# Attention probabilities times values cut in three parts of two key tiles instead of two parts of three

## The chip, the cores and the metric

The kernel runs on one core of a Trainium2 chip. The metric is the device time of one execution in microseconds. Runs of the kernel before gave 668.71, 668.14 and 669.58 us, median 668.71 us.

## The reference

The program is an attention with a hash mask, a Fourier mixing with a feed-forward block, and a gated convolution. The change touches the attention alone, and its last product:

```python
# q, k, v: 2 batches, 8 heads, 768 rows, head dimension 64; proj: 64 x 6
q_bucket = sum(((q @ proj) > 0) * powers);  k_bucket = sum(((k @ proj) > 0) * powers)
scores = where(q_bucket == k_bucket, q @ k.T / sqrt(64), -1e9)
attn = exp(scores - rowmax) / (rowsum + 1e-9)
x = attn @ v                          # <- the change is in the order of this product
u = x + real(fft(fft(x, axis=1), axis=2))
y = u + relu(norm(u) @ w_ch1) @ w_ch2
out = (sigmoid(causal_conv(y)) * (y @ w_val)) @ w_out
```

## The kernel before

The attention takes the first two fifths of the execution, to about 260 us. It works on pairs of heads, eight of them (`NP`), numbered i. A pair has twelve slots (`SLOTS`), one for each tile of 128 query rows: slots 0 to 5 hold the six tiles of the pair's first head, slots 6 to 11 those of its second. Pair 0 and pair 7 are written out; pairs 1 to 6 are the body of a hardware loop; a further round, numbered 8, has no scores and finishes what pair 7 left. Every engine follows an order written out by hand, and semaphores tie the orders together. Nothing is scheduled at run time.

In each slot, TensorE (function `pair`, lines 1286 to 1326) does the following, in this order:

- `scores` (line 1243): four matmuls of 384 columns write one query tile's scores into two PSUM banks. They wait (line 1239) until ScalarE has done the exponential of the tile two slots earlier, because only two such buffers exist.
- "P": six transposes (line 1307) of the probabilities of the tile two slots earlier, in two halves P0 and P1. Each half goes to one of three scratch banks in turn, and waits until the use three before it has been drained.
- in some slots a task that prepares the operands of a later head: B in slots 1 and 7 (line 1199), C0 in 2 and 8, C1 in 4 and 10 (line 1205), or "O" in slots 3 and 6, three transposes of a finished output (line 1315).
- in the slots that the table `PV_SLOTS` (line 241) lists, one part of the product with the values, `p_times_v` (lines 1246 to 1263).

The product has two halves g of the query rows for each pair, and each half sums over six key tiles kt into PSUM bank 7, both heads side by side: head 0 writes partitions 0 to 63 and head 1 partitions 64 to 127. Each (kt, head) is one float32 matmul in the program and two MATMUL records, each with its own weight load, in the trace, so one key tile has four records. Before the first part of a half TensorE waits for the transposed probabilities, for the values and for the copy of the bank's previous contents (`outT_copied`). After the last part it signals `pv_done`; ScalarE then copies the bank (line 686), later drains of the transposed probabilities may overwrite them, and the next values are loaded.

On VectorE a slot has the minimum of the new scores (line 927), a drain of half of the transposes (line 342) and the preparation's drains (lines 915 to 920). On ScalarE it has the exponential (line 676), the other drain (line 342), the rounding of the next operands, and the copy of the output (line 686).

Of the kernel before, what the change touches and what calls it, by code (L numbers as in the profile page):

```python
# [6 lines left out]
def attention_fft_ffn_gate_kernel(nc, qT, kT, v, proj, w_ch1, w_ch2, w_val, conv_wT, w_out,  # L7
# [27 lines left out]
    HT = T // 2  # L35
# [16 lines left out]
    with ctx:  # L52
# [172 lines left out]
        def need(eng, semaphore, value):  # L225

            if not isinstance(value, int) or value > 0:
                eng.wait_ge(semaphore, value)
# [9 lines left out]
        OUT_SLOT = {3: 0, 6: 1}  # L238

        P1_BY_ACT = (9,)  # L240
        PV_SLOTS = {11: (0, 0), 1: (0, 1), 2: (1, 0), 4: (1, 1)}
        uses = []
        for s in range(SLOTS):
            uses += [(s, "P0"), (s, "P1")]
# [45 lines left out]
        def wait_drained(eng, i, use):  # L290

            need(eng, scratch_free[bank_of(i, use)], use_number(i, use))
# [900 lines left out]
        def _(pe):  # L1193
# [17 lines left out]
            def prepare(i, use):  # L1211
                h, nxt = head_of_task(i, use)
                wait_free(i, use)
                if use[1] == "B":

                    need(pe, q_scaled, operands(i + nxt, h) + 1)
                    op = bits(i, use, h)
                else:
                    if use[1] == "C0":

                        of_head = range(6) if use[0] < 6 else range(6, SLOTS)
                        wait_drained(pe, i, (0 if isinstance(i, int) and i < 0 else
                                             next(x for x in of_head if "B" in PREPARE.get(x, [])), "B"))
                    op = buckets(i, use)
                op.then_inc(scratch_full[bank_of(i, use)], 1)
# [21 lines left out]
            def p_times_v(i, g, part):  # L1247

                if part == 0:

                    tile = T + HT * (g + 1) - 1
                    j, s = (i, tile + 2) if tile + 2 < SLOTS else (i + 1, tile + 2 - SLOTS)
                    wait_drained(pe, j, (s, "P0"))
                    wait_drained(pe, j, (s, "P1"))
                    need(pe, v_loaded, 32 * (i + 1))

                    need(pe, outT_copied, i * 2 + g)
                for kt in range(HT * part, HT * part + HT):
                    for h in range(2):
                        op = pe.matmul(PS[h * D:(h + 1) * D, 7, 0:HALF], v_in[:, h, kt, :],  # L1260
                                       probT[h][:, kt, g * HALF:(g + 1) * HALF], start=(kt == 0), stop=(kt == T - 1))
                if part == 1:
                    op.then_inc(pv_done, 1)

            def sequence_step(b, t, blocks):
# [23 lines left out]
            def pair(i, last):  # L1289
                first = isinstance(i, int) and i == 0  # L1290
                for s in range(SLOTS):
# [5 lines left out]
                    for use in slot_tasks(i, s, last):  # L1297
# [19 lines left out]
                        else:  # L1317
                            prepare(i, use)
                    if s in PV_SLOTS:
                        g, part = PV_SLOTS[s]  # L1320
                        if s == SLOTS - 1:
                            if last < 2:
                                p_times_v(i, g, part)
                        elif not first:
                            p_times_v(i - 1, g, part)
# [325 lines left out]
```

## Time and profile before

| | |
|---|---|
| median of three runs | 668.71 us |
| the profiled execution's own time | 668.71 us |
| its span, first to last instruction | 667.0 us |
| TensorE matmul busy | 633.6 us, 95% |
| TensorE weight load busy | 512.9 us, 77% |
| VectorE busy | 362.5 us, 54% |
| ScalarE busy | 304.6 us, 46% |
| GpSimd busy | 250.3 us, 38% |
| matmuls of the product with the values (line 1260) | 384 records, mean 494 ns, 69.0 us |

Matmuls are pipelined: one begins long before the one ahead of it has ended, so durations of single matmuls can't be added. What a step costs is read from the starts of the steps: from the start of its first matmul to the start of the first matmul of the next.

### The profile page before, as it was taken

The page shows a single profiled execution, that of the slowest core. Times are in us where ns is not written, and L with a number is a line of the kernel's source. Part 1 is how long each engine was busy: PE and PEld are TensorE (multiplying, and loading weights), DVE is VectorE, ACT ScalarE, POOL GpSimd, SP SyncE. Part 2 cuts the span into 40 slices and gives each one's busy share as a digit, 9 for nine tenths or more (in the row PEclk, how much of TensorE's full clock was granted, in tenths as well). Part 3 has the DMA queues.
Part 4 walks back from the last instruction along what each step waited for, and adds up shares of the span by engine and source line. Part 5 has one row for each costly group of instructions (what it writes and reads, how often), then busy time and mean ns, then how long its engine had stood idle before and what let it go on. Part 6 is the DMA issues. An engine that isn't in the chain of part 4 may idle for free.

```text
span 667.0 us, 11293 instructions
## 1 busy us (share of the span) xinstructions
PE 633.6 (95%) x3810; PEld 512.9 (77%) x3810; DVE 362.5 (54%) x599; ACT 304.6 (46%) x586; POOL 250.3 (38%) x202
## 2 busy tenths in 40 slices
PE   2999999999999999889999999999999999996998
PEld 1667666766767676888888888889888888885786
DVE  2878796877878786986111111116333333279720
ACT  2877676868677673465222222233222222251132
POOL 6643333335343243744233333326444444343140
PEclk9999999999999999989999999999999999998899
DMA  5822231323222000100222222511222221000102
GB/s 126 247 76 77 66 94 48 105 73 104 71 71 71 1 24 1 49 1 1 63 64 63 63 63 63 189 64 32 63 63 63 63 63 47 1 0 1 63 32 94
DMA packets 34263, 42.08 MB, mean 63 GB/s; under 512 B 3521, under 2 KB 22209, under 8 KB 34241
## 3 DMA queue, kind: packets, MB, share of 16 engines
q1 hardware_dynamic: 32512, 37.77, 19.4%
q0 software_dynamic: 1728, 4.02, 2.3%
q8 instruction: 14, 0.23, 0.2%
q14 instruction: 9, 0.07, 0.0%
HBM read 38.63 MB, written 3.15 MB: 63 GB/s over the span
## 4 chain that ended last, share of the span: by engine, by line
PE 82%; DVE 11%; issue 3%; POOL 2%; ACT 1%; DMA 1%; SPq 0%; DVEq 0%; POOLq 0%; ACTq 0%
PE banks L1457 20%; PE banks L1445 20%; PE banks L1260 10%; PE banks L1243 10%; PE banks L1307 7%; PE banks L1552 5%; PE banks L1199 2%; DVE row_min L927 2%; PE banks L1536 2%; DVE x_then_u_then_gate L1135 2%; PE banks L1380 2%; PE banks L1432 1%; DVE x_then_u_then_gate L1132 1%; DVE k_b L920 1%; PE banks L1283 1%
## 5 line engine op out<-in xcount | busy, mean ns | idle before, releaser
L1122 DVE SCALAR_TENSOR_TENSOR h_lo<-banks,h_hi 128x512 fp32r<-128x512 f32 x64 | 35.5, 558 | 180.8 <-ACT h_hi L825 180.8
L927 DVE TENSOR_REDUCE row_min<-banks 128x1 f32<-128x768 f32 x96 | 91.2, 956 | 42.2 <-PE banks L1243 41.7
L676 ACT ACTIVATE prob<-banks,row_min 128x768 f32<-128x768 f32 x96 | 87.1, 907 | 30.3 <-DVE row_min L927 30.3
L1445 PE MATMUL banks<-unT_hi,w_hi 128*128 128x512 f32 (+1 forms) x256 | 86.3, 337 | 0.0
L1445 PE MATMUL banks<-unT_hi,w_lo 128*128 128x512 f32 (+1 forms) x256 | 86.2, 337 | 0.0
L1445 PE MATMUL banks<-unT_lo,w_hi 128*128 128x512 f32 (+1 forms) x256 | 86.1, 336 | 0.0
L1307 PE MATMUL banks<-ident,prob 128*128 128x128 f32 x576 | 79.6, 274 | 2.2 <-DVE probT L342 1.3
L1307 PEld LDWEIGHTS banks<-ident,prob 128*128 128x128 f32 x576 | 67.2, 140 | 9.8 <-ACT probT L342 2.6
L563 POOL TENSOR_TENSOR w_lo<-w_stage,w_hi 128x512 fp32r<-128x512 f32 x32 | 43.5, 1361 | 83.0 <-ACT w_hi L741 83.0
L501 POOL TENSOR_TENSOR k_b<-k_raw,k_a 64x768 fp32r<-64x768 f32 x16 | 29.1, 1820 | 120.5 <-ACT k_a L659 120.5
L825 ACT ACTIVATE h_hi<-banks 128x512 fp32r<-128x512 f32 x64 | 31.2, 491 | 89.5 <-PE banks L1445 89.5
L568 POOL TENSOR_TENSOR w_lo<-w_stage,w_hi 128x512 fp32r<-128x512 f32 x32 | 41.6, 1302 | 79.4 <-ACT w_hi L746 79.4
L1260 PE MATMUL banks<-probT,v_in 128*64 128x384 f32 x384 | 69.0, 494 | 0.7 <-ACT outT L686 0.7
L1457 PE MATMUL banks<-h_hi,w_lo 128*128 128x512 f32 (+1 forms) x256 | 65.9, 339 | 0.0
L1457 PE MATMUL banks<-h_hi,w_hi 128*128 128x512 f32 (+1 forms) x256 | 65.9, 339 | 0.0
L1457 PE MATMUL banks<-h_lo,w_hi 128*128 128x512 f32 (+1 forms) x256 | 65.3, 337 | 0.0
L746 ACT CAST w_hi<-w_stage 128x512 fp32r<-128x512 f32 x32 | 19.9, 622 | 98.4 <-PE banks L1457 98.4
L1243 PE MATMUL banks<-k_a,q_a 128*128 128x384 f32 x192 | 59.1, 389 | 6.0 <-ACT prob L676 3.1
L342 ACT COPY probT<-banks 128x384 f32<-128x384 f32 x104 | 49.0, 481 | 32.2 <-PE banks L1307 31.2
L1135 DVE SCALAR_TENSOR_TENSOR x_then_u_then_gate<-x2T,taps,x_then_u_then_gate (+1 forms) x64 | 56.3, 879 | 5.3 <-DVE x_then_u_then_gate L1135 2.7
L1243 PEld LDWEIGHTS banks<-k_a,q_a 128*128 128x128 f32 x192 | 29.3, 191 | 34.1 <-ACT prob L676 21.2
L1445 PEld LDWEIGHTS banks<-unT_hi,w_hi 128*128 128x128 f32 x256 | 48.1, 188 | 6.7
(148 smaller groups left out, 1223.5 us busy)
## 6 DMA issues: line engine op xcount, KB each, us to landing
w_stage<-in_moe_w_ch SPq DMA_DIRECT2D x64, 256.0 KB, 2.9
q_raw<-in_q SPq DMA_DIRECT2D x32, 192.0 KB, 3.3
k_raw<-in_k SPq DMA_DIRECT2D x32, 192.0 KB, 3.6
v_in<-in_v SPq DMA_DIRECT2D x16, 192.0 KB, 2.4
out<-y_out SPq DMA_DIRECT2D x12, 256.0 KB, 2.0
seq_tables_sb<-in_dft POOLq DMA_DIRECT2D x6, 386.0 KB, 3.7
wvo_stage<-in_moe_w_val SPq DMA_DIRECT2D x1, 1024.0 KB, 5.3
wvo_stage<-in_moe_w_out SPq DMA_DIRECT2D x1, 1024.0 KB, 7.8
```

Source lines behind the costliest of these rows:

```text
L342: copy(dst, src).then_inc(scratch_free[bank_of(i, use)], 1)
L563: pool.tensor_tensor(w1_lo[:, slot, :, :], w1_stage[:, slot, :, :], w1_hi[:, slot, :, :].bitcast(F32), ALU.subtract).then_inc(w1_lo_done, 1)
L568: pool.tensor_tensor(w2_lo[:, slot, :], w2_stage[:, slot, :], w2_hi[:, slot, :].bitcast(F32), ALU.subtract).then_inc(w2_lo_done, 1)
L676: act.activation(prob[s % 2][:, :, :], s_tile(s), ACT.Exp, bias=row_min[:, s:s + 1], scale=-1.0, accum_out=row_sum[:, s:s + 1]).then_inc(e ...
L927: dve.tensor_reduce(row_min[:, s:s + 1], s_tile(s), AX.XY, ALU.min).then_inc(min_ready, 1)
L1122: dve.scalar_tensor_tensor(out=h_lo[:, slot, at:at + size], in0=h_bank[c], scalar=0.0, in1=h_hi[:, slot, at:at + size].bitcast(F32), op0=A ...
L1135: dve.scalar_tensor_tensor(out=dst, in0=src, scalar=weight, in1=dst, op0=ALU.mult, op1=ALU.add).then_inc(conv_step, 1)
L1243: op = pe.matmul(s_tile(s)[:, c, :], lhs[:, rows], rhs[:, c * HALF:(c + 1) * HALF], start=start, stop=not start)
L1260: op = pe.matmul(PS[h * D:(h + 1) * D, 7, 0:HALF], v_in[:, h, kt, :], probT[h][:, kt, g * HALF:(g + 1) * HALF], start=(kt == 0), stop=(kt ...
L1307: op = pe.transpose(bank[:, j * P:(j + 1) * P], prob[tile % 2][:, c, j * P:(j + 1) * P], ident[:, :])
L1445: op = pe.matmul(h_bank[c], w_[:, slot, kb, :], x_[:, kb, at:at + size], start=(kb == 0 and m == 0), stop=(kb == KB - 1 and m == 2))
L1457: op = pe.matmul(acc(d, c), w_[:, slot, cols], h_[:, slot, at:at + size], start=False, stop=last, skip_group_check=True)
```

## The change

The table gives each half of the product three slots instead of two, and each part two key tiles (eight records) instead of three (twelve). The first part of a half and its last one are in the slots they were in before (11 and 1 for half 0, 2 and 4 for half 1); the middle part is in slot 0 or slot 3. For each pair the first part runs in slot 11 and the rest in the slots 0 to 4 of the next round.

```diff
-        PV_SLOTS = {11: (0, 0), 1: (0, 1), 2: (1, 0), 4: (1, 1)}
+        PV_SLOTS = {11: (0, 0), 0: (0, 1), 1: (0, 2), 2: (1, 0), 3: (1, 1), 4: (1, 2)}
...
-                for kt in range(HT * part, HT * part + HT):
+                for kt in (2 * part, 2 * part + 1):
                     for h in range(2):
                         op = pe.matmul(PS[h * D:(h + 1) * D, 7, 0:HALF], v_in[:, h, kt, :],
                                        probT[h][:, kt, g * HALF:(g + 1) * HALF], start=(kt == 0), stop=(kt == T - 1))
-                if part == 1:
+                if part == 2:
                     op.then_inc(pv_done, 1)
```

## Rows read from the trace of the kernel before

**Rows 1.** The page: PE's busy line, and the chain that ended last.

```profile
PE 633.6 (95%) x3810; PEld 512.9 (77%) x3810; DVE 362.5 (54%) x599; ACT 304.6 (46%) x586; POOL 250.3 (38%) x202
...
PE 82%; DVE 11%; issue 3%; POOL 2%; ACT 1%; DMA 1%; SPq 0%; DVEq 0%; POOLq 0%; ACTq 0%
```

**Rows 2.** The waits: who waited for whom, us in total, times, longest.

```profile
PEld banks L1243 <- ACT prob L676: 21.2, 40, 1.0
```

**Rows 3.** The timeline, PE alone: start us, us, operation, count, [idle before].

```profile
150.85 0.62 PE L1243 MATMUL banks<-k_a,q_a 128*128 128x384 f32 x2
...
152.51 0.61 PE L1243 MATMUL banks<-k_a,q_a 128*128 128x384 f32 x2
...
154.47 0.62 PE L1243 MATMUL banks<-k_a,q_a 128*128 128x384 f32 x2
...
156.65 0.62 PE L1243 MATMUL banks<-k_a,q_a 128*128 128x384 f32 x2 [0.37 <-ACT prob L676]
...
157.46 0.82 PE L1307 MATMUL banks<-ident,prob 128*128 128x128 f32 x6
158.21 2.16 PE L1260 MATMUL banks<-probT,v_in 128*64 128x384 f32 x12
160.29 0.62 PE L1243 MATMUL banks<-k_a,q_a 128*128 128x384 f32 x2
...
161.10 0.82 PE L1307 MATMUL banks<-ident,prob 128*128 128x128 f32 x6
161.67 0.60 PE L1243 MATMUL banks<-k_a,q_a 128*128 128x384 f32 x2
...
162.46 0.82 PE L1307 MATMUL banks<-ident,prob 128*128 128x128 f32 x6
...
166.08 0.62 PE L1243 MATMUL banks<-k_a,q_a 128*128 128x384 f32 x2
...
171.36 0.49 PE L1315 MATMUL banks<-ident,outT 128*128 128x128 f32 x3
171.60 0.60 PE L1243 MATMUL banks<-k_a,q_a 128*128 128x384 f32 x2
...
180.88 0.62 PE L1243 MATMUL banks<-k_a,q_a 128*128 128x384 f32 x2
```

**Rows 4.** The timeline, weight loads of one part of the product (slot 11).

```profile
158.20 0.20 PEld L1260 LDWEIGHTS banks<-probT,v_in 128*64 128x64 f32 x4 [0.17 <-issue]
...
158.58 0.14 PEld L1260 LDWEIGHTS banks<-probT,v_in 128*64 128x64 f32 x2 [0.18 <-issue]
...
158.90 0.14 PEld L1260 LDWEIGHTS banks<-probT,v_in 128*64 128x64 f32 x2 [0.18 <-issue]
```

**Rows 5.** The timeline at the attention's end, where no scores remain.

```profile
247.32 2.16 PE L1260 MATMUL banks<-probT,v_in 128*64 128x384 f32 x12
...
251.00 2.16 PE L1260 MATMUL banks<-probT,v_in 128*64 128x384 f32 x12
...
255.91 0.55 PE L1315 MATMUL banks<-ident,outT 128*128 128x128 f32 x3
...
256.39 2.16 PE L1260 MATMUL banks<-probT,v_in 128*64 128x384 f32 x12
```

**Rows 6.** The timelines of DVE and ACT, slots 0, 1 and 5.

```profile
161.30 0.96 DVE L927 TENSOR_REDUCE row_min<-banks 128x1 f32<-128x768 f32 x1 [1.22 <-PE banks L1243]
...
176.43 0.96 DVE L927 TENSOR_REDUCE row_min<-banks 128x1 f32<-128x768 f32 x1 [0.90 <-PE banks L1243]
...
166.33 0.48 ACT L686 COPY outT<-banks 128x384 f32<-128x384 f32 x1
```

**Rows 7.** Windows: length, busy by engine (PE, PEld, DVE, ACT, POOL), clock, DMA share, GB/s.

```profile
287.90:291.30 3.40, 1.59 (x13) 1.34 (x12) 2.70 (x9) 3.40 (x9) 0.94 (x2) 1.00 0.00 0
291.30:294.70 3.40, 3.40 (x18) 3.40 (x17) 2.41 (x9) 1.19 (x3) 0.25 (x1) 0.50 0.00 0
...
612.20:622.40 10.20, 6.24 (x14) 4.46 (x15) 9.95 (x14) 1.66 (x2) 4.08 (x2) 0.50 0.00 0
```

## The prediction

> **What bounds the kernel now.** I read the page's first part and the chain of waits first: PE is busy for 95% of the span and carries 82% of the chain that ended last [rows 1]. The reader should ask next whether that holds inside the attention, where the change is. The total of waits says nearly: the only large wait of PE there is for ScalarE's exponential, 21.2 us in 40 waits of the weight load [rows 2], much of it hidden behind matmuls still running.
>
> Then I laid PE's timeline out by slots, for one pair in the steady loop [rows 3]. Scores of slot 8 start at 150.85 and those of the next pair's slot 8 at 180.88, so a pair takes 30.03 us. Slot 0 has scores and transposes alone and takes 161.67 - 160.29 = 1.38 us; that is what PE needs when nothing is late. Slot 9 has the same work and takes 154.47 - 152.51 = 1.96 us, so 0.58 us of waiting; slot 10 has the one matmul of C1 besides and takes 156.65 - 154.47 = 2.18 us, with 0.37 us of plain idle time at its end. Together they exceed 2 x 1.38 by 1.38 us, C1's matmul included, and that is the upper bound of PE's waiting in a pair. From slot 11 to slot 4, where the parts of the product are, PE runs on its own work: slot 11 takes 3.64 us, and its steps, priced below, add up to 3.64. So there an instruction added to PE, or a gap between two kinds of instruction, lengthens the pair by its whole length, unless slots 9 and 10 give it back.
>
> **The change, part by part.** No matmul is added or removed: 384 records before and after. What changes is how often PE enters and leaves a part of the product, and which slots are long.
>
> *The price of one part.* The part in slot 11 starts at 158.21 and the scores after it at 160.29: 2.08 us for twelve records [rows 3]. Its weight loads come in pairs, one for each head, every 158.90 - 158.58 = 0.32 us [rows 4]; six steps of 0.32 are 1.93 (0.3225 before rounding). The other 0.15 us is fixed: a slower first step (158.20 to 158.58 is 0.05 more than a step) and a slower exit. A part of eight records has four steps, 4 x 0.3225 + 0.15 = 1.44 us. So one cut into three parts instead of two costs 0.15 us more.
>
> *The price of entering.* Six transposes with scores behind them take 161.67 - 161.10 = 0.57 us to the next start; with the product behind them they take 158.21 - 157.46 = 0.75 us [rows 3]. That is 0.18 us more, and the weight loads show why: the first load of the values starts only at 158.20, after an idle time of 0.17 us that nothing but issue explains [rows 4], while the part's matmuls start at 158.21. In slot 3 the product now stands behind the O transposes. Three of these take 171.60 - 171.36 = 0.24 us with scores behind them [rows 3], and 256.39 - 255.91 = 0.48 us with the product behind them [rows 5], a difference of 0.24, but the latter are themselves behind a part of the product, which slows their start. I take 0.175 again, with 0.24 as the upper end. And scores that follow a part of the product take 161.10 - 160.29 = 0.81 us, those that follow transposes 162.46 - 161.67 = 0.79: 0.02 more in slots 1 and 4.
>
> The Trainium skill, TensorEngine Tiling (Array Packing), section Key Properties, says that a change of tiling mode drains the TensorE. The product uses 64 columns of the array for each head and its neighbours use all 128, so this rule and the fixed prices in the rows agree, and it speaks against the change. Against it stands the Trainium skill's page TensorE: Matmul & The Clock Gate, section Step-by-step: what each phase is for: weight loads are pulled ahead of matmuls in flight, so the next part's weights would load under the transposes. The rows show that this does not happen at the entry into the product. By the drain rule the sum below stands; by the other it would be without its entries, 2.5 us less.
>
> *The sum for a round of slots 0 to 4, in pairs 1 to 7.* Slots 1, 2 and 4 each lose two steps, 3 x 0.645 = 1.94 us. Slots 0 and 3 each gain 1.44 + 0.175 + 0.02 = 1.64 us, together 3.27. Net +1.34 us.
>
> *Slot 11, in pairs 0 to 6:* two steps fewer, -0.645 us each.
>
> *Slot 11 of pair 7 and the last round, without scores.* From the part in slot 11 to the next one took 251.00 - 247.32 = 3.68 us, with twelve transposes between them [rows 5]. After, it is part, transposes, part, transposes: 1.44 + 0.75 + 1.44 + 0.75 = 4.38, and the third part has two steps fewer than the second had, so 4.38 - 0.645 = 3.73: 0.05 later. Half 1 has its middle part directly in front of its last one there, at no price. I take +0.1.
>
> Sum: 7 x 1.34 - 7 x 0.645 + 0.1 = 9.38 - 4.52 + 0.1 = **+4.96 us**, about 0.69 us for a steady pair.
>
> *What could cover it.* The waits of slots 9 and 10 could. They arise because slots 5 to 10 have no part of the product, so that PE is quick there and VectorE and ScalarE fall behind. Before slot 5 they have caught up: VectorE's minimum of slot 5 comes after an idle time of 0.90 us and waits for PE [rows 6]. After the change slot 4 is 0.645 - 0.02 = 0.62 us shorter, so its scores come at most 0.62 us later, measured from slot 5. VectorE's idle time falls from 0.90 to no less than 0.28 us and stays above zero. So slots 5 to 10 start from the same state as before, with the same waits: nothing is given back, and nothing added.
>
> *New waits.* The middle parts wait for nothing; they read probabilities that slot 11's wait (or slot 2's) already covers. Three covers get thinner. First, the second half's first part, in slot 2, waits for ScalarE's copy of the first half's output. The copy starts at 166.33 [rows 6], 0.25 us after slot 2. Measured from slot 2, slot 1 starts 0.62 us later than before, so the copy ends at worst at 166.33 + 0.62 + 0.48 = 167.43; the part can't start before 166.08 + 0.81 + 0.75 = 167.64. It still fits. Second, slot 0's transposes need slot 11's drained. VectorE is done with those at 161.30 - 1.22 = 160.08 [rows 6]; the transposes come at 161.10 before and 161.10 - 0.645 = 160.46 after. It fits by 0.38 us. Third, the scores of slots 1 and 4 come later after the scores ahead of them, not sooner, so their buffers are free. If a cover is gone all the same, the cost is what it lacks, some 0.3 us a pair. I take zero.
>
> **Forecast.** The profiled execution's span of 667.0 becomes 672.0, and its time of 668.71, which is also the median of the runs, becomes 673.7 us.
>
> **Rivals.**
>
> *The waits in slots 9 and 10 give it back and more (faster).* If ScalarE and VectorE went into slot 5 with a lead that they lack now, the waits of at most 1.38 us a pair would shrink. All of it gone: 7 x (0.69 - 1.38) = -4.8 us, 663.9 us. It decides from the point where a pair's stretch from slot 5 to slot 11 becomes over 0.69 us shorter. For it: product work is now spread evenly over six slots. Against: the waits come five slots later, and both engines idle for PE at slot 5 already. Chance 0.04.
>
> *No entry price.* If the load of V's weights went under the transposes in the new places, 7 x 0.35 = 2.5 us would be gone: 671.2 us. With the fixed 0.15 as well hidden, 7 x 2 x 0.15 more: 669.1, which is no change. Against both: all the parts that follow transposes show the same prices. Chances 0.08 and 0.05.
>
> *A new wait in slots 0 to 4.* If a drain or ScalarE's copy comes late by 0.3 us in each of seven rounds, +2.1 us: 675.8 us. Chance 0.10.
>
> *The clock.* The granted clock fell to 0.50, the lower level of 1.2 GHz, at 291.3 us after PE had been busy for only 1.59 of 3.40 us, and again at 612.2 [rows 7]. The first stage costs up to 3.4 / 2 = 1.7 us, the second up to half of its 6.24 us of busy PE, 3.1 us. Both lie behind the attention, at places where PE waits anyway. The change shifts them by 5 us but not the work around them. This can move the time by -1.7 to +1.7 us in any case and is in the range, not in the sum.
>
> **How the numbers follow.** The forecast holds 0.73. Its own range is 7 x 0.6 to 7 x 0.8 us, so 672.9 to 674.3, and 672.3 to 675.2 with the spread that the runs of before have around their median (-0.57 and +0.87 us). To leave no more than 2 in 10 out I take 671.2 to 675.8, from the case without entry prices to the one with a new wait. A difference of 0.2%, 1.3 us, is about what a measurement of this kernel can tell from none. Slower by more than that: 0.73 + 0.08 + 0.10 = 0.91, less 0.01 for clock stages that hide it, 0.90; within: 0.06; faster: 0.04.
>
> **What would show each step.** In the changed profile a part of the product has eight records and goes from its start to the next scores in 1.44 us; slots 0 and 3 take about 3.0 and 3.3 us; transposes before the product in slot 0 take 0.75 us; a steady pair takes 30.7 us; PE's waits for the exponential stay near 21 us in total, in slots 9 and 10. The prediction is wrong if a pair takes 30.0 us or less, if transposes go into the product in 0.57 us in slot 0, or if a wait stands before the product in slots 0 to 4.

## Result and the profile after

The changed kernel took 672.52 us (median of five runs, 671.90 to 674.57) against 668.71 (five runs, 667.41 to 669.63). The ratio is 1.0065 with a 95% interval of 1.0045 to 1.0085: 3.0 to 5.7 us slower. The forecast of 673.7 us is a ratio of 1.0075, inside it. Three more runs of the changed kernel took 671.84, 673.57 and 673.81 us; with them its median is 673.05. The profiled execution has a span of 672.3 us, 5.3 more than before, and is one of the longer ones.

The page after: PE's busy line, the chain by engine, and the group of the product. The last two numbers of a group are busy time and mean ns, then the idle time ahead of it.

```profile
PE 638.7 (95%) x3810; PEld 512.0 (76%) x3810; DVE 364.8 (54%) x599; ACT 307.5 (46%) x586; POOL 250.7 (37%) x202
...
PE 81%; DVE 11%; issue 3%; POOL 2%; ACT 1%; DMA 1%; SPq 0%; DVEq 0%; POOLq 0%; ACTq 0%
...
L1260 PE MATMUL banks<-probT,v_in 128*64 128x384 f32 x384 | 72.3, 498 | 0.7 <-ACT outT L686 0.7
```

The same 3810 matmuls, and PE counts 5.1 us more as busy. So on this page the loss looks like work. It is not: the product's records have the same shortest, median and longest duration in both traces (486, 486 and 537 ns), and there are only more of the long ones, at the start of a part. Their mean rises from 494 to 498 ns. Only the starts show the loss. The timeline of PE alone after the change, from slot 11 to slot 5 (start, us, operation, count), answers to [rows 3]:

```profile
154.19 0.62 PE L1243 MATMUL banks<-k_a,q_a 128*128 128x384 f32 x2
...
159.97 0.62 PE L1243 MATMUL banks<-k_a,q_a 128*128 128x384 f32 x2 [0.37 <-ACT prob L676]
...
160.77 0.82 PE L1307 MATMUL banks<-ident,prob 128*128 128x128 f32 x6
161.52 1.51 PE L1260 MATMUL banks<-probT,v_in 128*64 128x384 f32 x8
162.96 0.62 PE L1243 MATMUL banks<-k_a,q_a 128*128 128x384 f32 x2
...
163.77 0.82 PE L1307 MATMUL banks<-ident,prob 128*128 128x128 f32 x6
164.52 1.51 PE L1260 MATMUL banks<-probT,v_in 128*64 128x384 f32 x8
165.96 0.62 PE L1243 MATMUL banks<-k_a,q_a 128*128 128x384 f32 x2
...
172.92 0.62 PE L1243 MATMUL banks<-k_a,q_a 128*128 128x384 f32 x2
...
174.38 0.49 PE L1315 MATMUL banks<-ident,outT 128*128 128x128 f32 x3
174.80 1.51 PE L1260 MATMUL banks<-probT,v_in 128*64 128x384 f32 x8
176.24 0.62 PE L1243 MATMUL banks<-k_a,q_a 128*128 128x384 f32 x2
...
184.88 0.44 PE L1243 MATMUL banks<-k_a,q_a 128*128 128x384 f32 x1
```

Slot 8 to slot 8 is 184.88 - 154.19 = 30.69 us, against 30.03. A part takes 162.96 - 161.52 = 1.44 us, and slot 0 takes 165.96 - 162.96 = 3.00 us, 1.62 more than before. In it the transposes lead into the product in 0.75 us. In slot 3 the O transposes lead into it in 174.80 - 174.38 = 0.42 us, 0.18 more than into scores, and that slot takes 3.32 us. No wait stands ahead of any part.

VectorE's minimum of slot 5, ScalarE's copy, and the total of PE's waits for the exponential, which answer to [rows 6] and [rows 2]:

```profile
180.42 0.96 DVE L927 TENSOR_REDUCE row_min<-banks 128x1 f32<-128x768 f32 x1 [0.47 <-PE banks L1243]
```
```profile
169.94 0.48 ACT L686 COPY outT<-banks 128x384 f32<-128x384 f32 x1 [0.26 <-PE banks L1260]
```
```profile
PEld banks L1243 <- ACT prob L676: 25.5, 46, 1.2
```

### The profile page after: what moved, and what is told of

It reads as the page before. It is cut to its first block, busy times and chain, and to the rows that moved or that the text cites. A ratio compares the mean times of both kernels' runs of the same rounds, so it can differ in the third digit from the quotient of the medians.

```text
span 672.3 us, 11293 instructions
## 1 busy us (share of the span) xinstructions
PE 638.7 (95%) x3810; PEld 512.0 (76%) x3810; DVE 364.8 (54%) x599; ACT 307.5 (46%) x586; POOL 250.7 (37%) x202
## 4 chain that ended last, share of the span: by engine, by line
PE 81%; DVE 11%; issue 3%; POOL 2%; ACT 1%; DMA 1%; SPq 0%; DVEq 0%; POOLq 0%; ACTq 0%
PE banks L1457 20%; PE banks L1445 20%; PE banks L1260 10%; PE banks L1243 10%; PE banks L1307 6%; PE banks L1552 5%; DVE row_min L927 2%; PE banks L1199 2%; PE banks L1536 2%; DVE x_then_u_then_gate L1135 2%; PE banks L1380 2%; PE banks L1432 1%; DVE x_then_u_then_gate L1132 1%; DVE probT L342 1%; DVE k_b L920 1%
## 5 line engine op out<-in xcount | busy, mean ns | idle before, releaser
L676 ACT ACTIVATE prob<-banks,row_min 128x768 f32<-128x768 f32 x96 | 87.0, 906 | 30.7 <-DVE row_min L927 30.7
L1260 PE MATMUL banks<-probT,v_in 128*64 128x384 f32 x384 | 72.3, 498 | 0.7 <-ACT outT L686 0.7
L1243 PEld LDWEIGHTS banks<-k_a,q_a 128*128 128x128 f32 x192 | 29.4, 192 | 42.7 <-ACT prob L676 25.5
```

The source lines that it names most:

```text
L676: act.activation(prob[s % 2][:, :, :], s_tile(s), ACT.Exp, bias=row_min[:, s:s + 1], scale=-1.0, accum_out=row_sum[:, s:s + 1]).then_inc(e ...
L1243: op = pe.matmul(s_tile(s)[:, c, :], lhs[:, rows], rhs[:, c * HALF:(c + 1) * HALF], start=start, stop=not start)
```

## Experiments

The theory: a steady pair grows by a price for each additional part of the product, paid where PE goes from matmuls 128 columns wide to matmuls 64 columns wide and back. The rivals: the loss comes from the shape of the slots (cover taken from slots 11 and 1), or from something else about the product, its float32 neighbours or its two matmuls side by side. For each kernel the period of a steady pair is read as in [rows 3], from slot 8 to slot 8; five such periods in one trace agree within 0.1 us, so a single profile measures 0.1 us a pair, which the times of whole runs could hardly. Where no ratio is given, each kernel was timed once, and the period carries the argument.

### Two uneven parts

```diff
-        PV_SLOTS = {11: (0, 0), 1: (0, 1), 2: (1, 0), 4: (1, 1)}
+        PV_SLOTS = {11: (0, (0, 1)), 1: (0, (2, 3, 4, 5)), 2: (1, (0, 1)), 4: (1, (2, 3, 4, 5))}
```

> Two parts a half in the slots of before (11, 1, 2, 4), but cut unevenly, two key tiles and then four (8 and 16 records instead of 12 and 12). Theory (a price of 0.15 us for each part and 0.18 us for each entry behind transposes, whatever the size): no part and no entry is added, so a steady pair takes 30.03 us as before and the time is that of before, 668.7 us within 0.2%; slot 11 takes 3.00 us instead of 3.64 and slot 1 takes 5.05 instead of 4.41. Rival (the loss came from shortening slots 11 and 1, whose length covered VectorE and ScalarE): part of the 0.65 us a pair shows up here, so 30.2 us or more and 670 us or more.

Measured: ratio 1.0006 to the kernel before (0.9996 to 1.0017), medians 668.60 against 667.99 us. Two starts of slot 8:

```profile
121.28 0.62 PE L1243 MATMUL banks<-k_a,q_a 128*128 128x384 f32 x2
...
151.29 0.62 PE L1243 MATMUL banks<-k_a,q_a 128*128 128x384 f32 x2
```

30.01 us a pair; slot 11 took 3.01 and slot 1 5.05 us. Slots 11 and 2 are as short here as in the changed kernel, and that costs nothing. Slots 1 and 4 are longer here, not shorter, so for them this run says nothing. The trace after the change does: the slots behind them, 5 to 10, take 1.38, 1.74, 2.34, 1.65, 1.97 and 2.16 us in the mean of five pairs, each within 0.01 us of before. The shape of the slots is not the cause.

### Half 0 alone in three parts

```diff
-        PV_SLOTS = {11: (0, 0), 1: (0, 1), 2: (1, 0), 4: (1, 1)}
+        PV_SLOTS = {11: (0, (0, 1)), 0: (0, (2, 3)), 1: (0, (4, 5)), 2: (1, (0, 1, 2)), 4: (1, (3, 4, 5))}
```

> Half 0 in three parts as in the changed kernel, half 1 in two parts as before. Theory: half the price, -0.645 in slot 11, -0.645 in slot 1, +1.64 in slot 0, so +0.34 us a pair, 30.37 us, and 668.7 + 7 x 0.34 = 671.1 us. Rival (one half alone pays, through ScalarE's copy of the output or a bank's drain): 30.03 or 30.7 us a pair.

Measured: 671.11 against 667.99 us, ratio 1.0043 (1.0026 to 1.0059).

```profile
122.42 0.62 PE L1243 MATMUL banks<-k_a,q_a 128*128 128x384 f32 x2
...
152.79 0.62 PE L1243 MATMUL banks<-k_a,q_a 128*128 128x384 f32 x2
```

30.37 us a pair: one additional part costs 0.34, about half of the 0.65 that two cost.

### A larger dose: four parts a half

```diff
+            PV_FIRST = (0, 3)        # here one key tile ahead of the transposes, one behind
+                    if s in PV_FIRST:
+                        product(i, s, last, first, slice(0, 1))
                     for use in slot_tasks(i, s, last):
...
+                    product(i, s, last, first, slice(1, 2) if s in PV_FIRST else slice(None))
```

> A larger dose: the changed kernel with the middle part of each half cut once more, one key tile ahead of the transposes of slot 0 or 3 and one behind them, so eight parts a pair instead of six. Theory: each further part costs 0.15 us for itself and 0.18 to 0.2 us for its entry, so about 0.35 us: 30.68 + 0.7 = 31.4 us a pair, and 7 x 0.7 = 5 us over the changed kernel. Rival (the change costs once, by its layout of slots, not by the part): 30.7 us.

Measured: 675.85 us, beside 668.67 for the kernel before. A start of slot 8, and slot 0 behind it:

```profile
124.51 0.62 PE L1243 MATMUL banks<-k_a,q_a 128*128 128x384 f32 x2
...
133.28 0.62 PE L1243 MATMUL banks<-k_a,q_a 128*128 128x384 f32 x2
134.18 0.87 PE L1260 MATMUL banks<-probT,v_in 128*64 128x384 f32 x4
134.97 0.87 PE L1321 MATMUL banks<-ident,prob 128*128 128x128 f32 x6
135.78 0.87 PE L1260 MATMUL banks<-probT,v_in 128*64 128x384 f32 x4
136.57 0.62 PE L1243 MATMUL banks<-k_a,q_a 128*128 128x384 f32 x2
```

A part of one key tile takes 134.97 - 134.18 = 0.79 us, of which 2 x 0.3225 = 0.645 is streaming: the same fixed 0.15. The pair takes 31.30 us in the mean, 0.31 for each further part, where 0.35 was expected. With four, five, six and eight parts a pair takes 30.03, 30.37, 30.68 and 31.30 us: the price is by the part.

### Middle parts ahead of the transposes

```diff
+            PV_FIRST = (0, 3)        # here the whole part stands behind the scores
+                    if s in PV_FIRST:
+                        product(i, s, last, first)
                     for use in slot_tasks(i, s, last):
...
-                    if s in PV_SLOTS:
+                    if s not in PV_FIRST:
+                        product(i, s, last, first)
```

> The changed kernel, but in slots 0 and 3 the product's part stands directly behind the scores and ahead of the transposes, so that it is entered from a fp32r matmul of 128 columns instead of from transposes. Theory (any step between 64-column and 128-column use has the price, whatever stands there): a steady pair takes 30.68 us as in the changed kernel, within 0.1. Rival (the entry price belongs to transposes ahead of the product): 2 x 0.175 less, 30.33 us.

Measured: 672.33 us, beside 668.67. Slot 0 of one pair:

```profile
161.89 0.62 PE L1243 MATMUL banks<-k_a,q_a 128*128 128x384 f32 x2
...
162.79 1.51 PE L1260 MATMUL banks<-probT,v_in 128*64 128x384 f32 x8
164.23 0.87 PE L1321 MATMUL banks<-ident,prob 128*128 128x128 f32 x6
164.86 0.59 PE L1243 MATMUL banks<-k_a,q_a 128*128 128x384 f32 x2
```

Scores lead into the product in 0.90 us instead of 0.81 into transposes, and transposes behind the product take 0.63 instead of 0.57. Together with the fixed 0.15 that is 0.30 a part instead of 0.34, and 30.63 us a pair (mean), not the 30.33 of the rival. The price hardly depends on what is next to the product.

### The same layouts with matmuls 128 columns wide

In both kernels the following stands in place of the product. It leaves out the pairing of each head's probabilities with that head's values: one head's probabilities (`kt % 2`) meet the values of two neighbouring key tiles. The parts and slots are those of the changed kernel and of the kernel before.

```diff
-                    for h in range(2):
-                        op = pe.matmul(PS[h * D:(h + 1) * D, 7, 0:HALF], v_in[:, h, kt, :],
-                                       probT[h][:, kt, g * HALF:(g + 1) * HALF], start=(kt == 0), stop=(kt == T - 1))
+                    op = pe.matmul(PS[:, 7, 0:HALF], v_in[:, kt % 2, min(kt, T - 2):min(kt, T - 2) + 2, :].rearrange("p t d -> p (t d)"),
+                                   probT[kt % 2][:, kt, g * HALF:(g + 1) * HALF], start=(kt == 0), stop=(kt == T - 1))
```

> The slots and the three parts of the changed kernel, but every key tile is one matmul with a stationary operand of 128 columns (64 values of two neighbouring key tiles) instead of two matmuls of 64 columns side by side; the values of the product are not those of the reference. A step still streams 384 columns in float32, so a key tile should take 0.645 us as before. Theory (the fixed prices belong to the change between 64-column and 128-column use of the array): the part of two key tiles takes 1.29 to 1.33 us instead of 1.44, transposes lead into it in 0.57 instead of 0.75 us, and the pair is within 0.1 us of the same layout with two parts. Rival (the prices belong to any change from transposes to a float32 product, or to leaving a float32 product): 1.44 and 0.75 us stay, and three parts cost 0.65 us more than two.

> The same wide matmuls in the two parts and slots of before, for comparison with the three-part one; the values of the product are not those of the reference. Theory: the pair is 4 x 0.15 + 0.18 = 0.8 us shorter than before, 29.2 us, less what slots 9 and 10 and the loss of cover give back. Rival: 30.0 us as before.

Measured: 657.78 us with three parts a half, 659.14 with two, one run each, beside 667.99 for the kernel before. The starts of slot 8 with two parts, and then slot 11 with three:

```profile
117.41 0.62 PE L1243 MATMUL banks<-k_a,q_a 128*128 128x384 f32 x2
...
146.20 0.62 PE L1243 MATMUL banks<-k_a,q_a 128*128 128x384 f32 x2
```
```profile
123.35 0.82 PE L1306 MATMUL banks<-ident,prob 128*128 128x128 f32 x6
124.00 1.46 PE L1259 MATMUL banks<-probT,v_in 128*128 128x384 f32 x4
125.00 0.81 PE L1243 MATMUL banks<-k_a,q_a 128*128 128x384 f32 x2
125.99 0.82 PE L1306 MATMUL banks<-ident,prob 128*128 128x128 f32 x6
```

The pair takes 28.79 us with two parts (28.80 in the mean) and 28.76 with three. More parts cost nothing here. The expectation erred in how the price would vanish: entry falls to 0.65 us, not 0.57, and from the part's start to the scores it is 1.00 us, not 1.3, but the scores behind it then take 0.99 instead of 0.81. From the transposes' start to the next slot's transposes it is 125.99 - 123.35 = 2.64 us, where the 64-column form of the changed kernel has 163.77 - 160.77 = 3.00: 0.36 us a part. It also undershot the whole: two parts a half save 1.23 us a pair, not 0.8.

The saving is not the same for every part. In slot 1 the part stands behind B, whose matmuls (line 1199) are 32 columns wide in every one of these kernels. The changed kernel first, and then the wide one with three parts:

```profile
166.78 0.82 PE L1307 MATMUL banks<-ident,prob 128*128 128x128 f32 x6
167.53 0.52 PE L1199 MATMUL banks<-q_raw,w_q 128*32 128x384 f32 x2
...
170.55 0.82 PE L1307 MATMUL banks<-ident,prob 128*128 128x128 f32 x6
```
```profile
128.64 0.82 PE L1306 MATMUL banks<-ident,prob 128*128 128x128 f32 x6
129.39 0.52 PE L1199 MATMUL banks<-q_raw,w_q 128*32 128x384 f32 x2
...
132.26 0.82 PE L1306 MATMUL banks<-ident,prob 128*128 128x128 f32 x6
```

Transposes lead into B in 0.75 us in both, as they do into the 64-column product. So the entry in slot 1 is paid for B, whatever the product is, and from these transposes to the next ones the wide kernel saves only 3.77 - 3.62 = 0.15 us. Read in the same way in the kernels with two parts a half, slot 1 saves 0.15 us and slots 11, 2 and 4 save 0.34 to 0.36 each, 1.20 of the 1.23 in all.

The weight loads in the wide kernel, beside those of [rows 4]:

```profile
123.18 0.75 PEld L1306 LDWEIGHTS banks<-ident,prob 128*128 128x128 f32 x6
123.89 0.95 PEld L1259 LDWEIGHTS banks<-probT,v_in 128*128 128x128 f32 x4
```

The first load for the product starts at 123.89, right behind the last of the transposes and 0.11 us ahead of the product's own first matmul at 124.00. The 64-column form starts its load 0.01 us ahead of the matmul and after 0.17 us of idle time.

### One of the two matmuls alone

```diff
-                    for h in range(2):
+                    for h in ((0, 1) if kt == 0 else (0,)):
...
-                                       probT[h][:, kt, g * HALF:(g + 1) * HALF], start=(kt == 0), stop=(kt == T - 1))
+                                       probT[h][:, kt, g * HALF:(g + 1) * HALF], start=(kt == 0), stop=(kt == T - 1 or h == 1))
```

> The changed kernel, but only the first key tile of a half has both heads' matmuls; the other five have head 0's alone, so the second head's product is left out but for one key tile. The matmuls stay 64 columns wide, but in slots 0, 1, 3 and 4 two neighbours are no longer side by side in the array. A record alone should take the 0.32 us that a pair takes, as in the wide kernels, so the length of the part is unchanged. Theory (the price belongs to the width of 64 columns among neighbours of 128): in slot 0 the transposes still lead into the part in 0.75 us, the part of four records takes 1.44 us, and a steady pair 30.7 us. Rival (the price belongs to two matmuls running side by side, which the wide kernels also lacked): 0.65 and about 1.3 us, and 28.8 to 29.3 us a pair.

Measured: 674.04 us, beside 668.11. Slot 0:

```profile
133.15 0.82 PE L1307 MATMUL banks<-ident,prob 128*128 128x128 f32 x6
133.89 1.50 PE L1260 MATMUL banks<-probT,v_in 128*64 128x384 f32 x4
135.33 0.62 PE L1243 MATMUL banks<-k_a,q_a 128*128 128x384 f32 x2
```

Entry 0.74 us (0.75 elsewhere), the part 1.44 us, a pair 30.66 us in the mean. With 160 of the product's 384 records left out, nothing is gained. The price belongs to the narrow width, not to two matmuls side by side or to their number.

### Fewer parts

Two kernels, each with one of these tables:

```diff
+        PV_SLOTS = {11: (0, (0, 1, 2)), 1: (0, (3, 4, 5)), 3: (1, (0, 1, 2, 3, 4, 5))}                     # half 1 whole
...
+        PV_SLOTS = {1: (0, (0, 1, 2, 3, 4, 5)), 2: (1, (0, 1, 2)), 4: (1, (3, 4, 5))}                      # half 0 whole
```

> Half 0 in two parts as before, half 1 in one part of 24 records in slot 3 (instead of slots 2 and 4). Theory of prices alone: one part less is -0.15 us, two entries behind C0 and C1 (0.09 each above scores) go and one behind O (0.175) comes: -0.15 us a pair, 29.9 us. Rival (fewer, longer parts leave VectorE and ScalarE late in the slots that lost theirs): new waits of PE ahead of slots 4 to 6, and 30.2 us or more.

> Half 0 in one part of 24 records in slot 1 behind B, none in slot 11; half 1 as before. Prices alone: one part and one entry behind transposes less, -0.34 us a pair, 29.7 us. But VectorE comes out of slot 10 with a backlog that it works off until 2.3 us into slot 11's product, and slots 11 and 0 would both be short; I expect PE to wait about 1 us in slots 0 and 1, so 30.3 to 30.7 us a pair, that is slower than before. Rival (cover does not matter, prices alone decide): 29.7 us and a faster kernel.

Measured: 680.34 and 675.55 us, beside 668.67; 31.65 and 31.07 us a pair. What PE waited for, in total, times and longest, with half 1 whole and then with half 0 whole (before: 2.8 us and 1.3 us in two waits each, all at the attention's start and end):

```profile
PE banks L1243 <- DVE k_b L920: 8.7, 9, 2.3
...
PE banks L1315 <- DVE k_b L920: 4.4, 7, 0.7
```
```profile
PE banks L1307 <- DVE probT L342: 4.6, 10, 1.1
```

With half 1 whole, PE waits for VectorE's drains of the preparation: 0.6 us in slot 3 ahead of the O transposes and 0.9 us ahead of slot 6's scores. The 29.9 us of the prices alone is refuted, and the rival, 30.2 us or more with new waits, holds. With half 0 whole, slots 11 and 0 take 0.51 and 0.85 us more than 1.38. That is 1.36 us lost against the 0.34 of prices saved, where I had expected 1 us in slots 0 and 1 and at most 30.7 us a pair. In slot 0 the transposes wait for VectorE's drain; what the loss in slot 11 waits for, the profile does not name. So cover does matter in both kernels with a whole half, though not down to the two parts a half that the kernel before has.

### The part in slot 11 ahead of the transposes

```diff
+            PV_FIRST = (11,)         # two parts a half, as before
```

> The kernel before, with the part in slot 11 directly behind the scores and ahead of the transposes. The middle parts put there cost 0.30 us around them instead of 0.34 in an earlier run (30.62 against 30.68 us a pair for two of them), so by the prices alone a pair takes 30.03 - 0.04 = 29.99 us and the time stays within 0.3 us of before, which can't be told from it. Rival (cover decides): slot 11's transposes come 2 us later, their drains then end close ahead of slot 0's second half of transposes, and PE waits there: 30.1 to 30.5 us a pair, up to 3 us slower.

Measured: 669.13 against 668.47 us, ratio 1.0008 (0.9998 to 1.0017); 30.00 us a pair in the mean. The 0.03 us a pair is 0.2 us in all and can't be told from nothing in the time. The rival, 30.1 to 30.5 us a pair, is refuted. This was the one version to which the experiments pointed as possibly better than both, and it is not shown to be.

## Why the prediction was right

- *The bound.* PE's own work in slots 11 to 4 sets the pace there: every gap added to PE appears in full in the pair. Shown by the dose (four, five, six, eight parts) and by slots 5 to 10, which kept their lengths.
- *The price of one part*, 0.15 us: 1.44 us for eight records, as forecast, and 0.79 for four.
- *The price of entering*, 0.175 us in slots 0 and 3: 0.18 measured in both. The O transposes behaved as the P ones, so the upper end of 0.24 was not needed.
- *The sum for a steady pair.* Forecast +0.69, measured +0.65 (30.68 against 30.03). Slot 0 gave 1.62 and slot 3 1.61 of the 1.64 forecast. Times seven that is 0.3 of the 1.15 us between forecast (+4.96) and medians (+3.81). The rest is within the interval of the measurement. The two traces come closer: from slot 8 of pair 0 to the first matmul behind the last part, 30.77 to 258.48 us before and 31.48 to 263.96 after, the change costs 4.77 us. In the last round it cost 0.16 us where 0.1 was forecast.
- *What could cover it.* VectorE's idle time at slot 5 fell from 0.90 to 0.47 us and stayed above zero, inside the bound of 0.28. Slots 9 and 10 took 1.97 and 2.16 us, as before. Nothing was given back.
- *The clock.* It was put in the range and not in the sum, and nothing came of it. Both stages at the lower level of 1.2 GHz are still there, with a granted clock of 0.51 from 296.5 to 299.9 us and from 617.5 to 627.7 us. Behind the attention the execution takes 408.3 us instead of 408.5.
- *No new waits.* ScalarE's copy now waits for the product, and not for its own list; it starts at 169.94, 0.19 us behind slot 2's start, and delays nobody.
- *A miss in the signs:* PE's weight loads waited 25.5 us for the exponential in 46 waits, not 21.2 in 40 [rows 2]. The matmuls' own idle time for it is 3.1 us in both traces, so the 4.3 us were hidden behind running matmuls. The total that I had named as a sign does not measure a loss.
- *A misreading of slot 1.* The prediction has all neighbours of the product at 128 columns. In slot 1 the neighbour is B, 32 columns wide, and the entry is paid there already. The sum did not suffer, since the change neither adds nor removes a part there.
- *The two rules of the Trainium skill.* TensorEngine Tiling (Array Packing), Key Properties, has a change of tiling mode drain the engine. The wide kernels and the one with head 0's matmuls alone show that the price is there with 64 columns and gone with 128, and B in slot 1 that 32 columns have the same entry. That a drain is the mechanism was not seen as such, only its price and its condition. TensorE: Matmul & The Clock Gate, Step-by-step: what each phase is for, has weight loads pulled ahead of matmuls in flight, on conditions of row groups or weight buffer that no run here tested: true here between matmuls of one width (0.11 us ahead, in the wide kernel), not into the 64-column product. The prediction weighed them as alternatives; they hold side by side.

The traces' spans differ by 5.3 us, more than the 4.77 us of the change. Of the 5.3, 0.71 us is there before any changed code runs: slot 8 of pair 0 starts at 30.77 us before and at 31.48 after, and between 30.48 and 31.62 us over all twelve traces, whose code is the same up to there. This spread of 1.1 us was not looked into.

## What to carry to other kernels

Read the cost of a step from starts, not from busy time. Where TensorE sets the pace, gather matmuls of one array width: in this kernel each stretch of 64-column matmuls among 128-column ones costs some 0.3 us, with one, two, three or four key tiles in it. A stretch that stands directly behind narrow matmuls pays only half of that (0.15 us in slot 1). Cut such a stretch only where another engine's lateness costs more than that, and check this by where PE waits, since spreading work evenly was worth nothing here in slots without a wait.

## What was not expected of the hardware

- The price is 0.30 to 0.36 us for one stretch of 64-column matmuls between 128-column ones, paid even in the kernel before: with the product at 128 columns and the same streaming a pair took 28.80 us instead of 30.03, and the kernel about 9 us less.
- A stretch of 64-column matmuls directly behind 32-column ones costs 0.15 us, and transposes lead into 32 columns in the same 0.75 us as into 64.
- One record of a 64-column float32 matmul over 384 columns takes the same 0.32 us step alone as two of them side by side in different columns of the array (parts of 1.44 us with four and with eight records), and as one 128 columns wide (slot 11 takes 0.64 us more with six such records than with four).
